# Attention handed over to two dense layers: the last pair's half copies on ScalarE, the third pair's sums and splits moved

## The chip, the cores and the metric

One core of a Trainium2 chip runs the whole program. The metric is the device time of one execution in microseconds (us), as the median of several runs; lower is better. Engines: PE is TensorE (matmuls, PEld its weight loads), DVE is VectorE, ACT is ScalarE, POOL is GpSimd, SP is SyncE, whose queue issues nearly all DMAs.

## The reference

The computation is rotary attention over 4 batches of 8 heads (576 tokens, head size 64), followed by two dense layers on 2304 tokens with model width 512 and hidden width 2048.

```python
q_rot, k_rot = rotate(q), rotate(k)
scores = 1/sqrt(D) * q_rot @ k_rot.T
attn = exp(scores - max); attn = attn / (sum(attn) + 1e-9)
x = attn @ v                        # then heads side by side: 2304 x 512
h = x @ w_in;  g = s * relu(h)**2 + b;  x = g @ w_out
h = x @ w2_in; g = h * sigmoid(1.702 * h); out = g @ w2_out
```

Everything is float32. The kernel feeds PE with a high and a low part of each operand (hi is a rounded copy in the type fp32r, lo is what the rounding left), so each product is three matmuls: hi by hi, lo by hi, hi by lo.

## The kernel before, in words

**Attention.** The 32 heads are worked in 16 pairs. Each engine follows an order written out by hand (`PE_ORDER`, `ACT_ORDER`, `DVE_ORDER`, `POOL_ORDER`, `SP_ORDER`), in which a token such as `sum1@-1` means the job "sum", half 1, of the pair one behind the step. `program` walks through it. The values product `PV` (L714) of a head leaves its result in PSUM as two halves of 64 partitions, one from the high and one from the low part of V. ACT copies one half to the tile `O` (`evac`, L808) and DVE copies the other to `osum` (`half`, L906). POOL's `finish` (L527, L531, L534) adds the two and multiplies by `inv_row`, the inverse row sums, into `xT`. `inv_row` is a single buffer. SP fetches it for a pair from DRAM with three DMAs (`get_inv`, L450), and for the last pair, number 15, only when `x_done` says that pair 14 is finished. For pairs 14 and 15 `finish` runs inside the first step of the layers.

**Layers.** These run in 48 steps (windows) n, 24 for each layer; a step handles 256 hidden columns of one of three chunks of 768 tokens. The input product of a step uses a scheme of 7 block products (`product(n, k)`, L1093, k = 0 to 6), which needs sums of weight blocks (`w_sum`, four POOL additions, L1021, L1022, L1024 and L1026, into the single tile `wsum`) and of the tokens (`x_sum`, POOL). The sums and the raw weights are split: ACT rounds to `win_hi` (`win_high`, L1031 and L1032), POOL takes `win_lo` of the raw part (`win_low`, L1038), DVE that of the sums from step 2 on (`sums_low`, L1042). `wout_high` (ACT, L1253) and `wout_low` (POOL, L1048) split the weights of the output product. The output product of a step is `y_part` (L1121), in three parts for each of its two tiles a and b.

**Within step n.** PE runs products k = 0 to 6 of step n. Between them it puts output parts: behind k = 0, 1, 2 tile b of step n-2, behind k = 3, 4, 5 tile a of step n-1. The seven products share two PSUM banks in turn, so each waits until ACT or DVE has read the one two before it: ACT copies k = 0 to `P1` (`keep_first`, L1137), k = 2 to `U2` (L1226) and k = 3 to `P5` (L1235). DVE adds k = 1 (`block_11`, L1142), k = 4 (L1299, into `h_b`) and k = 5 (L1303, into `h_a`). k = 6 needs the DVE addition of k = 4. For the step before, ACT runs the activation (L1187) and rounds to `ga_hi` and `gb_hi` (L1192); DVE runs the square (L1265 and L1271) and the low parts `ga_lo` and `gb_lo` (L1310). Products k = 0 and 1 of step 0 already run inside attention.

**The order around the change.** Semaphores hold the data; within an engine the order of the program decides. `pool_window(0)` runs `win_low(1)`, `w_sum(2)`, `wout_low(0)`, `finish(14)`, `finish(15)`; `pool_window(1)` begins with `win_low(2)`. Product (2, 0) waits for `win_low(2)` and `sums_low(2)`; the first output part of step n waits for `wout_low(n)` and `ga_lo`. DVE ends attention with the low parts of the first tokens (`xc_lo`, L919) for k = 3 to 6 and then the two half copies of pair 15. ACT in step 0 copies `U2`, `P5`, and then runs `wout_high(0)`, whose raw weights come by a DMA that SP issues once all values products are done. In what follows "(n, k)" is product k of step n.

Of the kernel before, what the change touches and what calls it, by code (L numbers as in the profile page):

```python
# [30 lines left out]
def fused_kernel(nc, q, k, v, w1_in, w1_out, w_s, w_b, w2_in, w2_out,  # L31
# [129 lines left out]
    with outer:  # L161
# [170 lines left out]
        with ExitStack() as ctx:  # L332
# [537 lines left out]
            def attention_vector(dve):  # L870
# [30 lines left out]
                def half(p, h, _):  # L901

                    dve.wait_ge(pv_done, 2 * p + h + 1)
                    if h == 0:
                        need(dve, x_done, p - 1)
                    dve.tensor_copy(osum[p % 2][rows_of(h), :], row(banks("PV", p, h), 0)[rows_of(1 - h), :]).then_inc(half_done, 1)  # L906
# [28 lines left out]
                for n, (first, w) in enumerate(((0, 0), (0, 1), (NM + 1, 0), (NM + 1, 1))):  # L935
# [5 lines left out]
                program(DVE_FIRST, DVE_ORDER, {"max": rowmax, "maxT": rowmaxT, "lo": lo, "loQ": loQ, "loT": loT, "inv": invert, "sum": half,  # L941
                                    "klo": qk_low, "xc": x_low, "first": first_block})

        with ExitStack() as ctx:
# [189 lines left out]
            def keep_first(act, n):  # L1134
                need(act, dve_read, 3 * n - 2)
                act.wait_ge(product_done, 7 * n + 1)
                act.copy(P1[:], hps(n, 0)).then_inc(act_read, 1)  # L1137

            def block_11(dve, n):
                dve.wait_ge(act_read, 4 * n + 1)  # L1140
# [53 lines left out]
            def act_window(act, n):  # L1194
# [3 lines left out]
                if gates:  # L1198
                    act.wait_ge(product_done, 7 * n)
                    act_function(act, a_b[:, 0:N], hps(n - 1, 6), n - 1).then_inc(act_read, 1)  # L1200
                    act.wait_ge(sq_a, n)
                    need(act, y_a, n - 2)
                    g_high(act, ga_hi[(n - 1) % 2][:], a_a[:], n - 1).then_inc(g_hi_a, 1)
                if runs:
                    if n > 0:
                        keep_first(act, n)
                    if j == 0 and C > 0:
                        x_split(act, C, NOPS - 1, True)
                    if splits:
                        x_split(act, C + 1, 0, True)  # L1210
                    if 0 < n and n + 1 < WINDOWS:
                        win_high(act, n + 1)
# [10 lines left out]
                if runs:  # L1223
                    act.wait_ge(product_done, 7 * n + 3)
                    need(act, dve_read, 3 * n)
                    act.copy(U2[:], hps(n, 2)).then_inc(act_read, 1)  # L1226
                    if splits:
# [7 lines left out]
                    act.copy(P5[:], hps(n, 3)).then_inc(act_read, 1)  # L1235
                    if n == 0:
                        wout_high(act, n)
                    if splits:
                        x_split(act, C + 1, 3, True)
                        x_split(act, C + 1, 4, True)  # L1240
# [14 lines left out]
            def dve_window(dve, n):  # L1255
# [4 lines left out]
                if gates:  # L1260
# [3 lines left out]
                    else:  # L1264
                        dve.scalar_tensor_tensor(a_a[:], a_a[:], sb_sb[:, 0:1], a_a[:], ALU.mult, ALU.mult).then_inc(sq_a, 1)  # L1265
                    dve.wait_ge(act_read, 4 * n)
                    if second(m):
# [8 lines left out]
                if runs:  # L1276
# [4 lines left out]
                    if evacuates:  # L1281
                        evacuate(dve, C - 1, 1)
                    if n > 0:
                        block_11(dve, n)
                    if 2 <= n + 1 < WINDOWS:
                        sums_low(dve, n + 1)
# [3 lines left out]
                if runs:  # L1290
# [11 lines left out]
                    dve.wait_ge(product_done, 7 * n + 6)  # L1302
                    dve.tensor_tensor(h_a[:, N:CH], hps(n, 5), U2[:], ALU.add).then_inc(dve_read, 1)  # L1303
                    if splits:
                        x_split(dve, C + 1, 5, False)
# [6 lines left out]
            def pool_window(pool, n):  # L1312
# [3 lines left out]
                if C + 1 < 2 * NCH and 1 <= j <= 4:  # L1316
# [3 lines left out]
                    x_sum(pool, C + 1, j - 1)  # L1320
                if n + 2 < WINDOWS:
                    w_sum(pool, n + 2)
                wout_low(pool, n)
                if n == 0:
                    finish(pool, NPAIR - 2)
                    finish(pool, NPAIR - 1)
# [104 lines left out]
```

## Time and profile before

| what | us |
|---|---|
| median of 3 runs | 1076.78 (1075.91 to 1077.61) |
| the profiled execution, its own time | 1077.13 |
| its span, first to last instruction | 1075.2 |
| PE busy | 1043.3 (97% of the span) |
| DVE, ACT, POOL busy | 737.1, 634.5, 706.5 |
| TensorE clock granted, mean | 0.998 of full speed |

What lies around the span is 1077.13 less 1075.2, 1.9 us. Attention takes up to about 314 us from the start, the 48 steps the rest. Times in the trace are from the start of the span. A row of the timeline gives the start, the duration, the engine, the line and operation, the tile written and those read, and in brackets the idle time before it with what ended it. A matmul lasts longer than the distance to the next one, as they are pipelined.

### The profile page before, as it was taken

How to read it: one execution, taken by the hardware profiler on the slowest of the kernel's cores; microseconds unless marked ns; L12 is line 12 of the kernel's file. 1: busy time of each engine (PE TensorE's matmuls, PEld its weight loads, DVE VectorE, ACT ScalarE, POOL GpSimd, SP SyncE). 2: the span in 40 equal slices, each digit the busy share in tenths (PEclk: the TensorE clock that was granted, in tenths of full speed). 3: DMA queues.
4: the chain of work that ended last, by engine and by line, in shares of the span. 5: the costliest groups of instructions: out<-in, count | busy, mean ns of one | idle time of the engine just before them, and what ended most of it. 6: DMA issues, size and time to landing. Idle time of an engine off the chain costs nothing.

```text
span 1075.2 us, 17071 instructions
## 1 busy us (share of the span) xinstructions
PE 1043.3 (97%) x6234; PEld 962.3 (90%) x6234; DVE 737.1 (69%) x874; ACT 634.5 (59%) x1125; POOL 706.5 (66%) x586
## 2 busy tenths in 40 slices
PE   4899999999989999999999999999999999999998
PEld 4799999999988999999999999998888889888887
DVE  6888888889887757755586564875577555854542
ACT  4887878787865545654565454654456434654542
POOL 6878787878888856667556754766566675555420
PEclk9999999999999999999999999999999999999999
DMA  4555455554232221221212221221222422241101
GB/s 107 129 150 150 111 143 143 153 132 114 65 96 71 79 79 59 79 60 59 78 59 80 60 78 60 59 79 59 79 60 69 128 61 78 59 137 59 60 20 59
DMA packets 100613, 93.03 MB, mean 87 GB/s; under 512 B 15652, under 2 KB 78644, under 8 KB 100532
## 3 DMA queue, kind: packets, MB, share of 16 engines
q1 hardware_dynamic: 99408, 90.94, 29.6%
q8 instruction: 50, 0.82, 0.3%
q10 hardware_dynamic: 1124, 1.02, 0.3%
q14 instruction: 31, 0.25, 0.1%
HBM read 69.44 MB, written 4.79 MB: 69 GB/s over the span
## 4 chain that ended last, share of the span: by engine, by line
PE 83%; POOL 5%; DVE 5%; ACT 3%; DMA 2%; issue 1%; SPq 0%; ACTq 0%; POOLq 0%; DVEq 0%
PE psum L1121 37%; PE psum L1093 31%; PE psum L714 6%; PE psum L642 3%; PE psum L668 3%; ACT E L777 2%; DVE negmax L876 1%; DVE Xlo L886 1%; PE psum L744 1%; DVE osum L906 1%; DVE QK L929 1%; POOL win_lo L1038 1%; POOL xT L531 1%; DMA sin<-in_k_sin_dram 0%; POOL osum L527 0%
## 5 line engine op out<-in xcount | busy, mean ns | idle before, releaser
L1038 POOL TENSOR_TENSOR win_lo<-win_raw,win_hi 128x768 fp32r<-128x768 f32 x48 | 101.6, 2116 | 244.2 <-ACT win_hi L1032 244.2
L1093 PE MATMUL psum<-xc_hi,win_hi 128*128 128x384 f32 x672 | 226.7, 337 | 4.2 <-DVE h_b L1299 2.4
L1093 PE MATMUL psum<-xc_lo,win_hi 128*128 128x384 f32 x672 | 226.7, 337 | 0.0
L1093 PE MATMUL psum<-xc_hi,win_lo 128*128 128x384 f32 x672 | 226.1, 336 | 0.0
L1093 PEld LDWEIGHTS psum<-xc_hi,win_hi 128*128 128x128 f32 x672 | 126.8, 189 | 13.7 <-issue 3.8
L1093 PEld LDWEIGHTS psum<-xc_lo,win_hi 128*128 128x128 f32 x672 | 126.7, 189 | 8.2
L1048 POOL TENSOR_TENSOR wout_lo<-wout_raw,wout_hi 128x1024 fp32r<-128x1024 f32 x48 | 119.6, 2492 | 16.5 <-ACT wout_hi L1253 16.5
L1093 PEld LDWEIGHTS psum<-xc_hi,win_lo 128*128 128x128 f32 x672 | 126.8, 189 | 0.0
L777 ACT ACTIVATE E<-psum,negmax 128x576 f32<-128x576 f32 x128 | 94.6, 744 | 13.4 <-DVE negmax L876 13.3
L876 DVE TENSOR_REDUCE negmax<-psum 128x1 f32<-128x576 f32 x128 | 91.0, 751 | 14.1 <-PE psum L642 13.5
L1042 DVE TENSOR_TENSOR win_lo<-wsum,win_hi 128x1024 fp32r<-128x1024 f32 x46 | 95.1, 2068 | 4.2 <-ACT win_hi L1032 4.1
L1299 DVE TENSOR_TENSOR h_b<-psum,P 128x384 f32<-128x384 f32 x48 | 26.7, 556 | 101.0 <-PE psum L1093 101.0
L642 PE MATMUL psum<-QK,Q 128*128 128x320 f32 (+1 forms) x512 | 85.5, 307 | 9.7 <-ACT E L777 6.7
L886 DVE TENSOR_TENSOR Xlo<-psum,Xhi 128x512 fp32r<-128x512 f32 x128 | 82.7, 681 | 4.8 <-ACT Xhi L791 4.7
L642 PEld LDWEIGHTS psum<-QK,Q 128*128 128x128 f32 x512 | 71.0, 189 | 14.9 <-issue 6.8
L1303 DVE TENSOR_TENSOR h_a<-psum,U 128x384 f32<-128x384 f32 x48 | 26.7, 557 | 82.6 <-PE psum L1093 82.5
L1021 POOL TENSOR_TENSOR wsum<-win_raw 128x256 f32<-128x256 f32 x48 | 63.8, 1328 | 20.3 <-DVE win_lo L1042 18.8
L714 PE MATMUL psum<-Xhi,V 128*128 128x256 f32 (+1 forms) x256 | 70.2, 302 | 0.4 <-DVE XTlo L894 0.4
L668 PE MATMUL psum<-id_sb,E 128*128 128x128 f32 x512 | 70.1, 276 | 0.6 <-ACT E L777 0.3
L791 ACT CAST Xhi<-psum 128x512 fp32r<-128x512 f32 x128 | 69.3, 581 | 0.3 <-PE psum L668 0.2
L714 PE MATMUL psum<-Xlo,V 128*128 128x256 f32 (+1 forms) x256 | 69.5, 296 | 0.0
L1253 ACT CAST wout_hi<-wout_raw 128x1024 fp32r<-128x1024 f32 x48 | 50.6, 1055 | 28.8 <-PE psum L1121 26.2
(154 smaller groups left out, 2852.5 us busy)
## 6 DMA issues: line engine op xcount, KB each, us to landing
wout_raw<-in_moe_w_out_dram SPq DMA_DIRECT2D x48, 512.0 KB, 3.6
win_raw<-in_moe_w_in_dram SPq DMA_DIRECT2D x48, 256.0 KB, 2.8
win_raw<-in_moe_w_in_dram SPq DMA_DIRECT2D x96, 128.0 KB, 2.8
Q<-QK SPq DMA_DIRECT2D x60, 144.0 KB, 2.8
QK<-QK SPq DMA_DIRECT2D x30, 288.0 KB, 3.4
vraw<-in_v_dram SPq DMA_DIRECT2D x32, 128.0 KB, 2.5
raw<-in_q_dram SPq DMA_DIRECT2D x30, 128.0 KB, 2.9
raw<-in_k_dram SPq DMA_DIRECT2D x30, 128.0 KB, 2.7
```

What stands on the lines that cost most here:

```text
L642: mm = pe.matmul(ps[:, a:b], Q[h][p % 2][:, at:at + P], QK[h][p % 2][:, part, c:c + b - a], start=part == 0, stop=part == 1)
L668: mm = pe.transpose(ps[:, t * P:(t + 1) * P], E[p % 2][:, t, h, c:c + P], id_sb[:])
L714: mm = pe.matmul(ps[:, a:b], V[h][:, j, :, :].rearrange("p a d -> p (a d)"), x, start=j == 0 and n == 0, stop=j == NM and n == 1, skip_gro ...
L777: act.activation(E[p % 2][:, j, h, :], row(banks("S", p, h, j), h), ACT.Exp, bias=negmax[p % 2][:, c:c + 1], accum_out=sums[p % 2][:, c:c ...
L791: act.copy(Xhi[:, h, j, 0:MAIN], banks("X", p, h, j)).then_inc(et_hi, 1)
L876: dve.tensor_reduce(negmax[p % 2][:, c:c + 1], row(banks("S", p, h, j), h), AX_X, ALU.max, negate=True).then_inc(max_done, 1)
L886: dve.tensor_tensor(Xlo[:, h, j, 0:MAIN], banks("X", p, h, j), Xhi[:, h, j, 0:MAIN].bitcast(F32), ALU.subtract).then_inc(et_lo, 1)
L1038: pool.tensor_tensor(win_lo[m % 2][:, 0:3 * BLK], win_raw[m % 2][:, 0:3 * BLK], win_hi[m % 2][:, 0:3 * BLK].bitcast(F32), ALU.subtract).th ...
L1042: last = eng.tensor_tensor(win_lo[m % 2][:, 3 * BLK:7 * BLK], wsum[:], win_hi[m % 2][:, 3 * BLK:7 * BLK].bitcast(F32), ALU.subtract)
L1048: pool.tensor_tensor(wout_lo[m % 2][:], wout_raw[m % 2][:], wout_hi[m % 2][:].bitcast(F32), ALU.subtract).then_inc(wout_lo_done, 1)
L1093: mm = pe.matmul(hps(n, k), w[n % 2][:, at:at + P], x[k][:, t, :], start=k in FRESH and t == 0 and i == 0, stop=t == HK - 1 and i == 2, sk ...
L1121: mm = pe.matmul(yps(bank)[:, col:col + size], lhsT, rhs, start=first and col == 0 and i == 0, stop=last and i == 2, skip_group_check=True)
```

## The change

The half copies of pair 15 leave DVE: `half` returns at once for it, and a new `last_halves` has ACT copy both behind `P5` of step 0 and ahead of `wout_high(0)`. On POOL, `w_sum(2)` goes from ahead of `wout_low(0)` to behind it, still ahead of `finish(14)`. In step 1 only, ACT's `keep_first` goes ahead of `ga_hi`, `U2` (now in a function, `keep_third`) ahead of `gb_hi`, and `win_high(2)` from ahead of `gb_hi` to behind `P5`; DVE's `block_11` goes ahead of the square of tile b, and `sums_low(2)` from ahead of `gb_lo` to the end of the step. All other steps keep their order.

```diff
--- before.py
+++ after.py
@@ -900,6 +900,8 @@
 
                 def half(p, h, _):
 
+                    if p == NPAIR - 1:
+                        return
                     dve.wait_ge(pv_done, 2 * p + h + 1)
                     if h == 0:
                         need(dve, x_done, p - 1)
@@ -940,6 +942,13 @@
                 dve.wait_ge(scale_set, 1)
                 program(DVE_FIRST, DVE_ORDER, {"max": rowmax, "maxT": rowmaxT, "lo": lo, "loQ": loQ, "loT": loT, "inv": invert, "sum": half,
                                     "klo": qk_low, "xc": x_low, "first": first_block})
+
+            def last_halves(act):
+
+                p = NPAIR - 1
+                act.wait_ge(x_done, p - 1)
+                for h in range(2):
+                    act.copy(osum[p % 2][rows_of(h), :], row(banks("PV", p, h), 0)[rows_of(1 - h), :]).then_inc(half_done, 1)
 
         with ExitStack() as ctx:
             def sb(name, shape, dt=F32):
@@ -1136,6 +1145,11 @@
                 act.wait_ge(product_done, 7 * n + 1)
                 act.copy(P1[:], hps(n, 0)).then_inc(act_read, 1)
 
+            def keep_third(act, n):
+                act.wait_ge(product_done, 7 * n + 3)
+                need(act, dve_read, 3 * n)
+                act.copy(U2[:], hps(n, 2)).then_inc(act_read, 1)
+
             def block_11(dve, n):
                 dve.wait_ge(act_read, 4 * n + 1)
                 dve.wait_ge(product_done, 7 * n + 2)
@@ -1198,17 +1212,21 @@
                 if gates:
                     act.wait_ge(product_done, 7 * n)
                     act_function(act, a_b[:, 0:N], hps(n - 1, 6), n - 1).then_inc(act_read, 1)
+                    if n == 1:
+                        keep_first(act, n)
                     act.wait_ge(sq_a, n)
                     need(act, y_a, n - 2)
                     g_high(act, ga_hi[(n - 1) % 2][:], a_a[:], n - 1).then_inc(g_hi_a, 1)
                 if runs:
-                    if n > 0:
+                    if n > 1:
                         keep_first(act, n)
+                    if n == 1:
+                        keep_third(act, n)
                     if j == 0 and C > 0:
                         x_split(act, C, NOPS - 1, True)
                     if splits:
                         x_split(act, C + 1, 0, True)
-                    if 0 < n and n + 1 < WINDOWS:
+                    if 1 < n and n + 1 < WINDOWS:
                         win_high(act, n + 1)
                 if gates:
                     act.wait_ge(sq_b, n)
@@ -1221,9 +1239,8 @@
                 if evacuates:
                     evacuate(act, C - 1, 0)
                 if runs:
-                    act.wait_ge(product_done, 7 * n + 3)
-                    need(act, dve_read, 3 * n)
-                    act.copy(U2[:], hps(n, 2)).then_inc(act_read, 1)
+                    if n != 1:
+                        keep_third(act, n)
                     if splits:
                         x_split(act, C + 1, 2, True)
                     if evacuates:
@@ -1234,7 +1251,10 @@
                     act.wait_ge(product_done, 7 * n + 4)
                     act.copy(P5[:], hps(n, 3)).then_inc(act_read, 1)
                     if n == 0:
+                        last_halves(act)
                         wout_high(act, n)
+                    if n == 1:
+                        win_high(act, n + 1)
                     if splits:
                         x_split(act, C + 1, 3, True)
                         x_split(act, C + 1, 4, True)
@@ -1263,6 +1283,8 @@
                         dve.tensor_tensor(a_a[:], h_a[:], a_a[:], ALU.mult).then_inc(sq_a, 1)
                     else:
                         dve.scalar_tensor_tensor(a_a[:], a_a[:], sb_sb[:, 0:1], a_a[:], ALU.mult, ALU.mult).then_inc(sq_a, 1)
+                    if n == 1:
+                        block_11(dve, n)
                     dve.wait_ge(act_read, 4 * n)
                     if second(m):
                         dve.tensor_tensor(a_b[:, 0:N], hps(m, 6), a_b[:, 0:N], ALU.mult).then_inc(last_read, 1)
@@ -1280,9 +1302,9 @@
                         x_split(dve, C + 1, 0, False)
                     if evacuates:
                         evacuate(dve, C - 1, 1)
-                    if n > 0:
+                    if n > 1:
                         block_11(dve, n)
-                    if 2 <= n + 1 < WINDOWS:
+                    if 2 < n + 1 < WINDOWS:
                         sums_low(dve, n + 1)
                 if gates:
                     dve.wait_ge(g_hi_b, n)
@@ -1301,6 +1323,8 @@
                         x_split(dve, C + 1, 4, False)
                     dve.wait_ge(product_done, 7 * n + 6)
                     dve.tensor_tensor(h_a[:, N:CH], hps(n, 5), U2[:], ALU.add).then_inc(dve_read, 1)
+                    if n == 1:
+                        sums_low(dve, n + 1)
                     if splits:
                         x_split(dve, C + 1, 5, False)
 
@@ -1318,10 +1342,11 @@
                         pool.wait_ge(x_lo, NOPS * (C + 1) - POOL_OPS)
                         x_ready(pool, C + 1)
                     x_sum(pool, C + 1, j - 1)
-                if n + 2 < WINDOWS:
+                if 0 < n and n + 2 < WINDOWS:
                     w_sum(pool, n + 2)
                 wout_low(pool, n)
                 if n == 0:
+                    w_sum(pool, n + 2)
                     finish(pool, NPAIR - 2)
                     finish(pool, NPAIR - 1)
```

## Rows read from the trace of the kernel before

**Rows 1.** the page, the chain that ended last, by engine

```profile
PE 83%; POOL 5%; DVE 5%; ACT 3%; DMA 2%; issue 1%; SPq 0%; ACTq 0%; POOLq 0%; DVEq 0%
```

**Rows 2.** waits of PE from 346.3 us to the end

```profile
PE psum L1121 <- POOL wout_lo L1048: 0.2, 1, 0.2
```

**Rows 3.** the chain in order of time (start us, us, what)

```profile
335.20 1.81 POOL win_lo L1038
...
343.87 2.37 POOL wout_lo L1048
...
346.29 1.68 PE psum L1121 x9
```

**Rows 4.** timeline of POOL (start us, us, what, [idle before <-releaser])

```profile
317.16 1.26 POOL L1021 TENSOR_TENSOR wsum<-win_raw 128x256 f32<-128x256 f32 x1
...
321.27 2.37 POOL L1048 TENSOR_TENSOR wout_lo<-wout_raw,wout_hi 128x1024 fp32r<-128x1024 f32 x1
323.60 2.14 POOL L527 TENSOR_TENSOR osum<-osum,O 128x576 f32<-128x576 f32 x1
...
327.67 1.03 POOL L534 TENSOR_TENSOR xT<-osum,inv_row 128x64 f32<-128x64 f32 x1
328.67 1.41 POOL L527 TENSOR_TENSOR osum<-osum,O 128x576 f32<-128x576 f32 x1
333.63 1.30 POOL L531 TENSOR_TENSOR xT<-osum,inv_row 128x512 f32<-128x512 f32 x1 [3.55 <-DMA inv_row<-inv_dram]
```

**Rows 5.** timeline of ACT

```profile
315.08 0.64 ACT L808 COPY O<-psum 64x576 f32<-64x576 f32 x1
...
316.28 0.48 ACT L1235 COPY P<-psum 128x384 f32<-128x384 f32 x1
317.84 1.05 ACT L1253 CAST wout_hi<-wout_raw 128x1024 fp32r<-128x1024 f32 x1 [1.08 <-DMA wout_raw<-in_moe_w_out_dram]
```

**Rows 6.** timeline of DVE

```profile
315.25 2.59 DVE L919 TENSOR_TENSOR xc_lo<-xT,xc_hi 128x768 fp32r<-128x768 f32 x1
317.76 1.49 DVE L919 TENSOR_TENSOR xc_lo<-x_sums,xc_hi 128x768 fp32r<-128x768 f32 x1
319.27 1.54 DVE L906 COPY osum<-psum 64x576 f32<-64x576 f32 x2
320.85 0.56 DVE L1299 TENSOR_TENSOR h_b<-psum,P 128x384 f32<-128x384 f32 x1
...
322.78 1.67 DVE L1265 SCALAR_TENSOR_TENSOR a_a<-a_a,sb_sb 128x768 f32<-128x768 f32 x1 [0.91 <-ACT a_a L1187]
324.38 2.17 DVE L1271 SCALAR_TENSOR_TENSOR a_b<-a_b,sb_sb 128x768 f32<-128x768 f32 x1
326.48 2.04 DVE L1310 SCALAR_TENSOR_TENSOR ga_lo<-a_a,sb_sb,ga_hi 128x768 fp32r<-128x768 f32 x1
```

**Rows 7.** timeline of PE

```profile
321.55 0.48 PE L1093 MATMUL psum<-xc_hi,win_hi 128*128 128x384 f32 x1 [2.35 <-DVE h_b L1299]
...
325.27 0.34 PE L1093 MATMUL psum<-xc_hi,win_hi 128*128 128x384 f32 x1
...
326.31 0.33 PE L1093 MATMUL psum<-xc_hi,win_hi 128*128 128x384 f32 x1
...
329.04 0.45 PE L1093 MATMUL psum<-xc_hi,win_hi 128*128 128x384 f32 x1 [1.52 <-DVE h_a L1142]
...
330.21 0.40 PE L1121 MATMUL psum<-ga_hi,wout_hi 128*128 128x512 f32 x1
...
337.55 0.34 PE L1093 MATMUL psum<-xc_hi,win_hi 128*128 128x384 f32 x1
```

**Rows 8.** durations min/median/max ns, L1022 and L1271 (the columns end in first and last start)

```profile
L1022 POOL TENSOR_TENSOR wsum<-win_raw x47: 723/735/1452, 307.1 to 1020.5; 128x256 f32<-128x256 f32 x47
...
L1271 DVE SCALAR_TENSOR_TENSOR a_b<-a_b,sb_sb x24: 1005/1018/2175, 324.4 to 685.6; 128x768 f32<-128x768 f32 x24
```

**Rows 9.** PE, PEld, DVE, ACT, POOL busy, granted clock, DMA; between 321.5 and 329.0 us

```profile
321.50:329.00 7.50, 5.97 (x24) 5.68 (x24) 6.59 (x6) 6.15 (x10) 7.42 (x5) 0.77 0.00 0
```

## The prediction

> **What bounds the kernel now.** I read the chain that ended last first: PE holds 83% of it [rows 1]. Then the waits of PE behind 346.3 us: there is one in 729 us, of 0.2 us, for `wout_low(1)` [rows 2]. So whatever PE gains or loses by the start of the first output part of step 1, at 346.29 [rows 3], stays to the end, and the change is to be judged by that one moment. Next I asked what sets it. The chain in order of time has POOL work ahead of it: `win_low(2)` at 335.20, then an `x_sum`, `w_sum(3)` and `wout_low(1)`, which ends at 343.87 + 2.37 = 346.24 [rows 3]. `win_low(2)` starts when `finish(15)` ends, and that waited for `inv_row` up to 333.63 [rows 4]. That transfer is issued only when `finish(14)` is over, at 327.67 + 1.03 = 328.70 [rows 4]. POOL runs without a gap from 317.16 to there. PE on the other hand has waits between 319.2 and 329.0: 2.35 us for `h_b` and 1.52 us for `h_a` [rows 7]. They look like the thing to repair, but PE, repaired, meets the POOL chain. At 337.55 it starts (2, 0) [rows 7], only 0.54 us behind the end of `win_low(2)` at 335.20 + 1.81 = 337.01 [rows 3]: PE's slack against POOL there is half a microsecond.
>
> **Part 1, the half copies.** DVE loses two copies, 1.54 us at 319.27 [rows 6]. ACT gets them behind `P5`, which ends at 316.76. They read and write what one `evac` copy does, 64 x 576, so they cost at most 0.64 us each [rows 5], and begin one 0.55 us behind the other as neighbours here overlap a little: 316.8 to 317.95. ACT would otherwise sit idle for 1.08 us up to 317.84, for the DMA of `wout_raw` [rows 5]. So `wout_high(0)` slips by 0.1 us and ends at about 318.95 and not 318.89. Without that cover it would slip by 1.2 us. The new wait of ACT, for pair 13's `finish`, was met inside attention. `finish(15)` needs the halves far later than 318, so nothing waits.
>
> **Part 2, `w_sum(2)` behind `wout_low(0)`.** POOL is free at 317.05, but `wout_low(0)` needs `wout_high(0)`: it stands idle until 319.0, where before it had begun its four additions at 317.16. Behind the start the work up to the end of `finish(14)` is the same: `w_sum` 4 x 0.72, `wout_low` 2.37, `finish` 1.41 + 1.29 + 0.31, 8.3 us when nothing disturbs it (the 0.72 is the shortest of L1022 [rows 8], 2.37 and 1.41 are [rows 4], and the last two together are the 1.57 from 333.63 to 335.20 [rows 3, 4]). It took 328.70 - 317.16 = 11.54. The 3.3 us more go with DVE: in that stretch lie five DVE instructions with two SBUF inputs, at 315.25 (its end), 317.76, 322.78, 324.38 and 326.48, of 1.5 to 2.6 us each [rows 6] where such a one takes 1.01 alone [rows 8]. They interlock with POOL's. The one at 324.38 ends (326.55) 0.8 us behind the end of POOL's L527 (325.74), and POOL's next ones are long by 0.6 to 0.7 us each. That is 3.3 / 5 = 0.66 us of POOL per DVE instruction. After the change DVE has four of them beside this work (L1265, L1271, and L1310 for `ga_lo` and `gb_lo`; the low part at 317.76 now meets an idle POOL, takes about 0.95 us and ends near 318.7). Sum: 319.0 + 8.3 + 4 x 0.66 = 329.95 and not 328.70, **+1.3 us**. Bounds: with no such DVE instruction in the way 327.3 (-1.4), with the stretch as long as before, 319.0 + 11.54 = 330.5 (+1.8).
>
> The Trainium skill, page "SBUF — State Buffer", section "SBUF: two separate sides", says why: the port pair that DVE and GpSimd share is an exclusive lock held for the whole instruction, and the other engine blocks. The trace agrees with the 0.8 us above. By that rule one counts collisions; were it a division of bandwidth one would scale the stretch, and the sum would be 0.5 us larger.
>
> **Part 3, the transfer and `finish(15)`.** SP's three DMAs go out 1.3 us later, so `inv_row` is there at 333.63 + 1.3 = 334.9; SP's loads of later weights behind them slip as much, under the 11 us that POOL needs from one step to the next. DVE is by now 2 to 3 us ahead of its old times, so its L1271 and L1310 of step 2 fall upon `finish(15)`, which had taken its undisturbed 1.57 us: +0.66 to +0.8. `finish(15)` ends near 337.3 where it was 335.20: **+2.1 us**. `win_low(2)` ends at 339.1, and (2, 0) starts at 339.2 and not 337.55: +1.65.
>
> **Part 4, what PE and DVE gain, and why it is hidden.** `h_b` is no longer behind the copies: DVE ends it at 319.3, k = 6 of step 0 follows at once and not at 321.55, and the clock stays up. `block_11(1)` ahead of the square of tile b is done at 323.2, so (1, 3) need not wait. The square of tile b and `ga_lo` follow to about 325.7; the first output part starts at 325.8 where it was 330.21 [rows 7]. From there to (2, 0) PE needs 337.55 - 330.21 = 7.34 us, so it would want (2, 0) at 333.2. There it stands until 339.2, for 6 us. `win_high(2)` (1.8 us on ACT) starts with `w_sum(2)`, near 326.3, and is over before `h_b` of step 1 wants ACT at 329; `sums_low(2)` runs at 331.8 to 333. Neither sets a time. For `keep_first`, `keep_third` and `block_11` the cost is nothing: the same instructions, earlier, on engines that wait there.
>
> **Part 5, the clock.** After 2.35 us of idle PE the matmuls ran at half rate: the twelve from 321.55 took 325.27 - 321.55 = 3.72 us, and six at full rate take 326.31 - 325.27 = 1.04 [rows 7]; the granted clock of that stretch is 0.77 of full [rows 9], between the levels of 1.2 and 2.4 GHz. That spell cost 3.72 - 2.08 = 1.6 us. Before the 1.52 us gap at 329.04 PE was busy as well, and there the rate held. A gap of 6 us should bring the clock down again, and now on the path: **+1.6 us**. Bounds: 0 and, with the spell half as long again, 2.4.
>
> **Part 6, on to 346.29.** From (2, 0) to there PE took 346.29 - 337.55 = 8.74, of which 0.2 was the wait for `wout_low(1)`. POOL, from 339.1, needs `x_sum` 1.8, `w_sum(3)` 2.9 and `wout_low(1)` 2.4 undisturbed, to 346.2. PE comes later, so the 0.2 goes. **Sum: +1.65 + 1.6 - 0.2 = +3.1 us.** Against the profiled execution (span 1075.2 and 1.9 around it, 1077.13) that is 1080.2. The median is 0.35 lower, 1076.78, so I forecast 1079.9.
>
> **Rivals.** A measurement of this kernel can tell about 0.2% from no change, 2.15 us: 1074.6 and 1078.9 are the limits.
> *A, the forecast, 0.60:* `finish(14)` late, PE stands, the clock falls: +3.1; with the bounds above +2.0 to +4.5.
> *B, POOL late but the clock stays up or is back at once, 0.17:* +1.5 (1078.3), from +0.7 to +2.1. For it: most gaps here leave the rate as it was. Against it: the shorter one at 321.55 did not.
> *C, POOL meets one or two DVE instructions fewer, 0.13:* `win_low(2)` ends about where it did, PE starts (2, 0) at 337.5, and the result is 0 with the clock up, +1.4 with it down.
> *D, faster, 0.10:* the idle POOL and the empty DVE keep out of each other's way altogether. Then `finish(14)` ends at 327.3, `finish(15)` at 333.8, (2, 0) starts at 335.7 after a gap of 2.5 us, and `wout_low(1)` is there by 342.9: 335.7 - 337.55 - 0.2 = -2.1 to -2.5 us, 1074.5. It decides from the point at which `finish(14)` ends before 328.7; every microsecond before that is one off the end, unless the clock takes it back. Against it: three of the four DVE instructions depend on PE and ACT only, and fall into the same stretch.
> That the change doesn't do what it says I leave out: the new order on each engine is plain in the diff.
>
> **The numbers.** Slower by over 0.2%: nearly all of A (0.56), a little of B and C (0.05): 0.61. Faster: most of D, 0.08. The rest, 0.31, is within. The range goes from 1076.7, where C without the clock is still in, to 1081.5, the upper end of A with 0.05 left out; below lies D with a part of C. A's own range is 1078.8 to 1081.3.
>
> **What would show it.** Right: k = 6 of step 0 near 319.3; POOL idle for about 1.9 us ahead of `wout_low(0)`; L534 of `finish(14)` ending near 330; PE idle for some 6 us ahead of (2, 0), with the releaser POOL `win_lo`, and matmuls at half rate behind it; the first output part of step 1 near 349. Wrong: `finish(14)` ending before 328.7, (2, 0) before 337.5, or half rate nowhere behind 337.

## The result, and the profile after

The changed kernel takes 1080.41 us (median of 7 runs, 1079.19 to 1081.17) against 1076.78 before on the same chip. The ratio is 1.0031 with a 95% interval of 1.0019 to 1.0043: 3.6 us slower, where I had forecast 3.1 us and 1079.9. The profiled execution took 1080.41, its span is 1078.3 against 1075.2, 3.1 us more.

The PE timeline of the changed kernel (start us, us, what, in brackets the idle time before with its releaser) answers to [rows 7]. Lines behind the edits have moved by 2 to 24: the input product is L1102, the output product L1130.

```profile
319.74 0.41 PE L1102 MATMUL psum<-xc_hi,win_hi 128*128 128x384 f32 x1
...
326.50 0.48 PE L1130 MATMUL psum<-ga_hi,wout_hi 128*128 128x512 f32 x1 [1.29 <-issue]
...
339.40 0.69 PE L1102 MATMUL psum<-xc_hi,win_hi 128*128 128x384 f32 x1 [5.32 <-POOL win_lo L1047]
...
342.96 0.28 PE L1130 MATMUL psum<-gb_lo,wout_hi 128*128 128x256 f32 x1
...
349.51 0.39 PE L1130 MATMUL psum<-ga_hi,wout_hi 128*128 128x512 f32 x1
```

k = 6 of step 0 starts at 319.74 with no wait and not after 2.35 us. The first output part starts at 326.50, where it was 330.21. Then comes what the forecast turned on: (2, 0) stands for 5.32 us, released by POOL's `win_lo`, and the matmuls of 384 columns behind it are spaced 0.32 us and not 0.17. Full rate is back at 342.96. The first output part of step 1 starts at 349.51 and not 346.29. The clock, in the windows view (busy time of PE, PEld, DVE, ACT, POOL, then the granted clock), is at half, the level of 1.2 GHz:

```profile
329.00:337.50 8.50, 5.08 (x29) 4.36 (x27) 6.04 (x6) 2.80 (x4) 5.96 (x7) 0.92 0.33 96
337.50:341.00 3.50, 1.60 (x5) 1.60 (x6) 0.19 (x1) 0.00 (x0) 3.50 (x2) 0.50 0.14 37
```

The POOL timeline answers to [rows 4]:

```profile
319.67 2.40 POOL L1057 TENSOR_TENSOR wout_lo<-wout_raw,wout_hi 128x1024 fp32r<-128x1024 f32 x1 [2.23 <-ACT wout_hi L1273]
322.02 1.45 POOL L1030 TENSOR_TENSOR wsum<-win_raw 128x256 f32<-128x256 f32 x1
...
324.13 1.45 POOL L1033 TENSOR_TENSOR wsum<-wsum,win_raw 128x256 f32<-128x256 f32 x1
325.66 1.33 POOL L1035 TENSOR_TENSOR wsum<-win_raw,wsum 128x256 f32<-128x256 f32 x1
326.95 2.15 POOL L527 TENSOR_TENSOR osum<-osum,O 128x576 f32<-128x576 f32 x1
...
330.44 0.33 POOL L534 TENSOR_TENSOR xT<-osum,inv_row 128x64 f32<-128x64 f32 x1
...
334.61 1.28 POOL L531 TENSOR_TENSOR xT<-osum,inv_row 128x512 f32<-128x512 f32 x1 [2.46 <-DMA inv_row<-inv_dram]
...
336.83 2.51 POOL L1047 TENSOR_TENSOR win_lo<-win_raw,win_hi 128x768 fp32r<-128x768 f32 x1
...
343.96 2.42 POOL L1057 TENSOR_TENSOR wout_lo<-wout_raw,wout_hi 128x1024 fp32r<-128x1024 f32 x1
```

POOL waits 2.23 us for `wout_hi`, then has `wout_low(0)`, the four sums (322.02 to 326.95), `finish(14)` to 330.77, the transfer to 334.61, `finish(15)` to 336.87 and `win_low(2)` to 339.34. `wout_low(1)` ends at 346.38, 3 us ahead of PE. DVE and ACT over the same time answer to [rows 6] and [rows 5]:

```profile
318.18 0.95 DVE L921 TENSOR_TENSOR xc_lo<-x_sums,xc_hi 128x768 fp32r<-128x768 f32 x1
319.05 0.55 DVE L1321 TENSOR_TENSOR h_b<-psum,P 128x384 f32<-128x384 f32 x1
...
321.14 1.74 DVE L1285 SCALAR_TENSOR_TENSOR a_a<-a_a,sb_sb 128x768 f32<-128x768 f32 x1 [0.92 <-ACT a_a L1201]
...
323.68 1.31 DVE L1293 SCALAR_TENSOR_TENSOR a_b<-a_b,sb_sb 128x768 f32<-128x768 f32 x1
324.92 1.48 DVE L1334 SCALAR_TENSOR_TENSOR ga_lo<-a_a,sb_sb,ga_hi 128x768 fp32r<-128x768 f32 x1
326.32 1.49 DVE L1334 SCALAR_TENSOR_TENSOR gb_lo<-a_b,sb_sb,gb_hi 128x768 fp32r<-128x768 f32 x1
```

```profile
317.22 1.29 ACT L951 COPY osum<-psum 64x576 f32<-64x576 f32 x2
318.54 1.05 ACT L1273 CAST wout_hi<-wout_raw 128x1024 fp32r<-128x1024 f32 x1
```

Attention ended 0.44 us later in this execution than in the one of before (last values matmul at 314.21, before at 313.77). That is not the change: over the 13 profiles of this case, this matmul starts anywhere from 313.57 to 314.38. So that kernels can be compared, the table gives three moments counted from that matmul (the mark), in us: the end of `finish(14)`, the start of (2, 0) and the start of the first output part of step 1, and then the difference of the last to the kernel before. In the last column stands the median less that of the kernel before on the same chip, with the interval of the ratio. The moments are those of one profiled execution of each kernel, the medians are of all its executions. Most profiled executions lie within 0.5 us of their median, but that of E2 lies 0.95 us below it and that of E8 1.3 us above, as the slowest of its 11.

| kernel | `finish(14)` ends | (2, 0) | output, step 1 | to before | median to before (ratio, 95%) |
|---|---|---|---|---|---|
| before | 14.9 | 23.8 | 32.5 | | |
| after | 16.6 | 25.2 | 35.3 | +2.8 | +3.6 (1.0019 to 1.0043) |
| E1 halves alone | 15.3 | 23.5 | 32.7 | +0.2 | +0.9 (0.9997 to 1.0015) |
| E2 sums ahead | 15.7 | 24.2 | 33.4 | +0.9 | +2.0 (1.0007 to 1.0025) |
| E3 sums in the transfer | 12.9 | 23.1 | 31.6 | -0.9 | -0.5 (0.9988 to 1.0006) |
| E4 filler | 16.5 | 25.5 | 34.0 | +1.4 | +1.8 (1.0004 to 1.0021) |
| E5 halves back | 15.4 | 25.8 | 34.3 | +1.8 | +1.6 (1.0007 to 1.0024) |
| E6 pad | 18.5 | 26.6 | 36.7 | +4.1 | +4.7 (1.0031 to 1.0055) |
| E7 finish ahead | 7.6 | 21.6 | 30.7 | -1.8 | -1.2 (0.9977 to 0.9994) |
| E8 E7's move on the kernel before | 7.6 | 27.0 | 35.4 | +2.9 | +1.7 (1.0006 to 1.0023) |
| E9 finish in attention | 1.4 | 21.0 | 30.1 | -2.5 | -1.8 (0.9979 to 1.0003) |
| E10 E9's move on the kernel before | 1.4 | 25.1 | 33.4 | +0.9 | +0.9 (0.9996 to 1.0014) |
| E11 after, again | 16.6 | 25.2 | 36.3 | +3.8 | +4.1 (1.0023 to 1.0049) |

### The profile page after: what moved, and what is told of

Its sections match the earlier page's. It is cut to its first block, busy times and chain, and to the rows that moved or that the text cites. A ratio compares the mean times of both kernels' runs of the same rounds, so it can differ in the third digit from the quotient of the medians.

```text
span 1078.3 us, 17070 instructions
## 1 busy us (share of the span) xinstructions
PE 1045.1 (97%) x6234; PEld 963.6 (89%) x6234; DVE 730.4 (68%) x872; ACT 636.9 (59%) x1127; POOL 703.3 (65%) x586
## 4 chain that ended last, share of the span: by engine, by line
PE 85%; POOL 4%; DVE 4%; ACT 3%; issue 2%; DMA 1%; SPq 0%; ACTq 0%; POOLq 0%; DVEq 0%
PE psum L1130 37%; PE psum L1102 31%; PE psum L714 6%; PE psum L668 4%; PE psum L642 4%; ACT E L777 2%; DVE negmax L876 1%; PE psum L744 1%; DVE osum L908 1%; DVE Xlo L886 1%; POOL win_lo L1047 1%; POOL xT L531 0%; PE psum L678 0%; POOL osum L527 0%; PE psum L694 0%
## 5 line engine op out<-in xcount | busy, mean ns | idle before, releaser
L1102 PE MATMUL psum<-xc_hi,win_hi 128*128 128x384 f32 x672 | 226.4, 337 | 5.8 <-POOL win_lo L1047 5.3
L1102 PE MATMUL psum<-xc_lo,win_hi 128*128 128x384 f32 x672 | 226.2, 337 | 0.0
L1102 PE MATMUL psum<-xc_hi,win_lo 128*128 128x384 f32 x672 | 225.6, 336 | 0.0
L1102 PEld LDWEIGHTS psum<-xc_hi,win_hi 128*128 128x128 f32 x672 | 126.4, 188 | 15.3 <-POOL win_lo L1047 5.6
L1102 PEld LDWEIGHTS psum<-xc_lo,win_hi 128*128 128x128 f32 x672 | 126.5, 188 | 8.2
L1102 PEld LDWEIGHTS psum<-xc_hi,win_lo 128*128 128x128 f32 x672 | 126.4, 188 | 0.0
L777 ACT ACTIVATE E<-psum,negmax 128x576 f32<-128x576 f32 x128 | 94.7, 745 | 13.5 <-DVE negmax L876 13.3
L1051 DVE TENSOR_TENSOR win_lo<-wsum,win_hi 128x1024 fp32r<-128x1024 f32 x46 | 94.7, 2059 | 1.9 <-ACT win_hi L1041 1.7
```

The source lines that it names most:

```text
L777: act.activation(E[p % 2][:, j, h, :], row(banks("S", p, h, j), h), ACT.Exp, bias=negmax[p % 2][:, c:c + 1], accum_out=sums[p % 2][:, c:c ...
L1051: last = eng.tensor_tensor(win_lo[m % 2][:, 3 * BLK:7 * BLK], wsum[:], win_hi[m % 2][:, 3 * BLK:7 * BLK].bitcast(F32), ALU.subtract)
L1102: mm = pe.matmul(hps(n, k), w[n % 2][:, at:at + P], x[k][:, t, :], start=k in FRESH and t == 0 and i == 0, stop=t == HK - 1 and i == 2, sk ...
```

## The experiments

Theory: POOL's chain (`finish(14)`, transfer, `finish(15)`, `win_low(2)`) sets (2, 0); moving the sums behind `wout_low(0)` lengthened it, and the gap that PE's own gain opened brought the clock down on the path. Rivals: the steps moved on ACT and DVE are the cause, or there is no slack-free chain on POOL at all. Part 1 is, as in the prediction, the half copies on ACT, and part 2 the place of the sums on POOL. What is left of the change are the moves in step 1.

**E1, part 1 alone.** The kernel before, with `half` returning for the last pair and `last_halves` on ACT.

```diff
                 def half(p, h, _):
+                    if p == NPAIR - 1:
+                        return
...
                     if n == 0:
+                        last_halves(act)
                         wout_high(act, n)
```

> The kernel before with part 1 alone (half copies of pair 15 on ScalarE). POOL-chain theory: k = 6 of step 0 starts 1.5 to 2 us earlier and no longer at half rate, but POOL still begins its four additions near 317.2, finish(14) still ends near 328.7, and (2, 0) cannot start before win_low(2) ends near 337: the time is that of before within 1 us. Rival (the waits of PE for DVE set the end): 1.6 to 3 us faster than before.

Measured +0.9 us, not told from no change. The waits of PE show where the 2.35 us went (E1, PE timeline):

```profile
319.33 0.41 PE L1102 MATMUL psum<-xc_hi,win_hi 128*128 128x384 f32 x1 [0.64 <-DVE h_b L1309]
...
327.30 0.45 PE L1102 MATMUL psum<-xc_hi,win_hi 128*128 128x384 f32 x1 [2.96 <-DVE h_a L1151]
...
346.60 0.50 PE L1130 MATMUL psum<-ga_hi,wout_hi 128*128 128x512 f32 x1 [0.56 <-POOL wout_lo L1057]
```

The wait for `h_b` is 0.64 us and the rate holds behind it, but 2.96 us are now lost on `h_a` of `block_11(1)`, and half rate follows there from 328.9 on. PE then starts (2, 0) at 337.38, when `win_low(2)` has just ended (337.33), and ahead of 346.60 it waits 0.56 us for `wout_lo`. So part of what part 1 gains is lost in the next wait for DVE, and POOL takes the rest. The rival, a kernel 1.6 to 3 us faster, is out.

**E2, part 2 undone.** The changed kernel with the sums back ahead of `wout_low(0)`.

```diff
-                if 0 < n and n + 2 < WINDOWS:
+                if n + 2 < WINDOWS:
                     w_sum(pool, n + 2)
                 wout_low(pool, n)
                 if n == 0:
-                    w_sum(pool, n + 2)
                     finish(pool, NPAIR - 2)
```

> The changed kernel with the sums of the third pair back ahead of wout_low(0). POOL-chain theory: POOL's 2.2 us of idle go, finish(14) ends about 1.3 us earlier than in the changed kernel, (2, 0) starts 1 to 2 us earlier, behind a gap of about 4 us that still brings the clock down: 1 to 2 us faster than the changed kernel, still 0.5 to 2.5 us slower than before. Rival (the place of the sums on POOL is innocent, the loss comes from the steps moved on ScalarE and VectorE): the same as the changed kernel, some 3.5 us slower than before.

1078.95 us, +2.0 against +3.6 for the change: in the range of the theory, so the place of the sums accounts for nearly half of the loss. (The two intervals overlap a little. In the table `finish(14)` ends 0.9 us and (2, 0) starts 1.0 us earlier than in the changed kernel.) The rest comes with the steps that stayed moved: DVE's squares come earlier and fall upon `wout_low(0)`, which takes 3.12 us and not 2.37, and `finish(14)` still ends 0.7 us later than before. E2 is E1 with the moves in step 1, on the same chip, and takes 1.1 us more (0.7 in the table). So with part 1 in place these moves gain nothing. The difference is within the intervals, and no run undoes them alone in the changed kernel. The expectation had one thing wrong. The gap ahead of (2, 0) is 1.43 us, not 4, and the half rate lies elsewhere, behind the gap ahead of the first output part (E2, PE timeline and windows):

```profile
327.31 0.76 PE L1130 MATMUL psum<-ga_hi,wout_hi 128*128 128x512 f32 x1 [2.08 <-issue]
...
337.85 0.45 PE L1102 MATMUL psum<-xc_hi,win_hi 128*128 128x384 f32 x1 [1.43 <-POOL win_lo L1047]
```

```profile
327.00:331.00 4.00, 3.69 (x13) 3.44 (x14) 2.17 (x2) 2.08 (x4) 3.72 (x3) 0.57 0.07 13
```

There it costs PE time that POOL's chain hides, as (2, 0) still has to wait for `win_lo`.

**E3, the sums in the transfer.** The changed kernel with `w_sum(2)` between the two finishes.

```diff
                 if n == 0:
+                    finish(pool, NPAIR - 2)
                     w_sum(pool, n + 2)
-                    finish(pool, NPAIR - 2)
                     finish(pool, NPAIR - 1)
```

> The changed kernel with the sums of the third pair behind finish(14), in the time in which POOL waits for inv_row. POOL-chain theory: finish(14) ends near 326, inv_row lands near 331, finish(15) ends near 332.5, win_low(2) near 335, (2, 0) starts near 335 behind a gap of 1 to 2 us that leaves the clock up: about 2.5 us faster than before (1 to 3.5), 6 us faster than the changed kernel. Rival (ScalarE, held up by the later sums at win_high(2), is late with the activations of step 1 and takes the gain): no faster than before.

Against the changed kernel 4 us are won back, against before only 0.5, which is no difference: the main number was missed, and the time is the one that the rival gave. The POOL timeline says why:

```profile
319.84 2.40 POOL L1057 TENSOR_TENSOR wout_lo<-wout_raw,wout_hi 128x1024 fp32r<-128x1024 f32 x1 [2.22 <-ACT wout_hi L1273]
322.19 2.15 POOL L527 TENSOR_TENSOR osum<-osum,O 128x576 f32<-128x576 f32 x1
...
330.88 1.44 POOL L527 TENSOR_TENSOR osum<-osum,O 128x576 f32<-128x576 f32 x1
...
334.92 2.51 POOL L1047 TENSOR_TENSOR win_lo<-win_raw,win_hi 128x768 fp32r<-128x768 f32 x1
```

`finish(14)` now ends at 327.29, 12.9 behind the mark, but POOL has no wait left after 319.84: the transfer is hidden, and what sets (2, 0) is the plain amount of work between `wout_hi` and `win_low(2)`, 17.6 us with its collisions (`finish(14)` 5.1 us where it takes 3.0 undisturbed, `win_low(2)` 2.51 where it takes 1.85). I had left the collisions out of this expectation, though the prediction's own rule of 0.66 us each was at hand. ACT was indeed held for 3.5 us at `win_high(2)`, as the rival had it, but what released (2, 0) was POOL's `win_lo`, and the first output part of step 1 had no wait at all. So the rival's number came by another path.

**E4, PE kept busy in the gap.** Ahead of (2, 0) of the changed kernel:

```diff
+                if n == 2 and k == 0:
+                    pe.wait_ge(dve_read, 3 * n)
+                    for i in range(28):
+                        pe.matmul(hps(n, k), xc_hi[0][:, 0, 0:P], xc_hi[0][:, 0, :], start=True, stop=True, skip_group_check=True)
```

> The changed kernel with 28 idle matmuls of 384 columns (4.9 us at full rate) put into the gap ahead of (2, 0), into the PSUM bank that (2, 0) clears at its start. Theory that the half rate behind the gap is on the path: (2, 0) starts when it did, the matmuls behind it run at full rate, and the time is 1.4 to 1.8 us below that of the changed kernel. Rival (POOL's wout_low(1) or ScalarE would set the first output part of step 1 anyway): no gain, the wait comes back ahead of that part.

1078.79, 1.6 us below the changed kernel's first median, though in another set of runs (each against its own kernel before: +1.8 and +3.6); on the marks 35.3 - 34.0 = 1.3, with (2, 0) 0.3 later. E4's windows, from (2, 0) on (compare 337.50:341.00 above, clock 0.50):

```profile
339.40:348.00 8.60, 8.57 (x49) 8.04 (x50) 2.61 (x3) 4.35 (x6) 8.52 (x7) 1.00 0.31 70
```

Between (2, 0) and the output part lie 8.5 us here, 10.1 in the changed kernel. Eight of its 11 executions have a mean clock of 1.000. Work that computes nothing makes the kernel faster: the half rate behind the gap is on the path and costs 1.6 us.

**E5, part 1 undone.** The changed kernel with the half copies back on DVE (the diff of E1 reversed).

> The changed kernel with the half copies of pair 15 back on VectorE. POOL-chain theory: h_b and k = 6 of step 0 come some 1.3 us later than in the changed kernel, but wout_low(0) and the sums keep their place and (2, 0) starts within 1 us of 339, behind a gap of about 4 us instead of 5.3: the time is that of the changed kernel within 1 us (1079.5 to 1081.5). Rival (part 1 is worth its 1.5 us at the end too): 1.3 to 3 us slower than the changed kernel.

1078.35: 2 us *faster* than the changed kernel (1.0 us by the marks; the two intervals overlap a little), outside what both theories said. Two things show in the trace. POOL: ACT begins `wout_high(0)` 4.0 us behind the mark and not 4.3, and then DVE's first square, later by 1.5 us, meets POOL less: the four sums take 3.6 us and not 4.9 and `finish(14)` ends 1.2 us earlier. PE: with a gap of 1.80 us for `h_b` and one of 2.60 us ahead of the first output part (at 328.88) the clock falls at about 330, before (2, 0) and not behind it, and what then releases (2, 0) is DVE's `sums_low(2)`, which ends at 339.29, while `win_low(2)` was done at 336.41 (E5, DVE and PE):

```profile
336.41 2.88 DVE L1049 TENSOR_TENSOR win_lo<-wsum,win_hi 128x1024 fp32r<-128x1024 f32 x1
```

```profile
328.88 0.47 PE L1128 MATMUL psum<-ga_hi,wout_hi 128*128 128x512 f32 x1 [2.60 <-issue]
...
330.94 0.52 PE L1100 MATMUL psum<-xc_lo,win_hi 128*128 128x384 f32 x1
...
339.39 0.41 PE L1100 MATMUL psum<-xc_hi,win_hi 128*128 128x384 f32 x1 [1.39 <-issue]
```

So in the changed kernel part 1 is not worth nothing but costs: it brings DVE's work into POOL's, and it makes PE's gap one long one in the worst place.

**E6, POOL loaded.** The changed kernel with this ahead of `finish(14)`:

```diff
+        pad = keep("pad", [P, 768])
...
+                    for i in range(2):
+                        pool.tensor_tensor(pad[:, i * 384:(i + 1) * 384], win_raw[0][:, 0:384], win_raw[0][:, 512:896], ALU.add)
                     finish(pool, NPAIR - 2)
```

> The changed kernel with two additions of 384 elements on GpSimd (about 1.0 us each, into a tile of their own) ahead of finish(14). POOL-chain theory: they are on the path, finish(14), the transfer, win_low(2) and (2, 0) all slip by 2.0 us (1.3 to 2.7, as collisions with VectorE shift), and so does the time: about 1082.5. Rival (GpSimd has slack there): no change.

`finish(14)` ends 1.9 us later, (2, 0) and the output part 1.4 us later (by the marks), the median is 1081.52, 1.1 above the changed kernel's. The intervals overlap, but all five executions (1081.32 and more) lie above all 12 of the changed kernel (1081.25 at most, E11 included). Of the 1.9 us, 1.4 arrive and not all: `win_low(2)`, pushed away from DVE's work, takes 1.80 us and not 2.51. POOL is on the path; the rival is out. Its gap (E6, PE timeline):

```profile
340.49 0.69 PE L1103 MATMUL psum<-xc_hi,win_hi 128*128 128x384 f32 x1 [6.65 <-POOL win_lo L1048]
```

**E7, `finish(14)` where POOL sat idle.** The changed kernel with

```diff
+                if n == 0:
+                    finish(pool, NPAIR - 2)
                 wout_low(pool, n)
                 if n == 0:
                     w_sum(pool, n + 2)
-                    finish(pool, NPAIR - 2)
                     finish(pool, NPAIR - 1)
```

> The changed kernel with finish(14) ahead of wout_low(0), where GpSimd sat idle; the sums stay behind wout_low(0). POOL-chain theory: the transfer of inv_row is over before finish(15) wants it, GpSimd works without a gap from 317 to win_low(2), 13.1 us of undisturbed work and some 5 us of collisions, (2, 0) starts near 335.3 behind a short gap with the clock up: 2.0 to 2.8 us faster than before, near 1074.6. Rival (collisions on the port now delay VectorE's last xc_lo and take it back on TensorE): no faster than 1 us below before.

1075.61, 1.2 us below before (interval 0.6 to 2.5), 5 us below the changed kernel. Less than the theory's 2.0 to 2.8 and just beyond the rival's 1: both have a share. (2, 0) starts 2.1 us earlier than before, near the 335.3 that I gave (335.64, with attention 0.2 us later); but DVE's last `xc_lo` takes 2.18 us beside `finish(14)` and not 0.95, so PE waits 1.35 us for `h_b` (E7, DVE and PE):

```profile
317.99 2.18 DVE L921 TENSOR_TENSOR xc_lo<-x_sums,xc_hi 128x768 fp32r<-128x768 f32 x1
```

```profile
320.78 0.41 PE L1102 MATMUL psum<-xc_hi,win_hi 128*128 128x384 f32 x1 [1.35 <-DVE h_b L1321]
...
335.64 0.41 PE L1102 MATMUL psum<-xc_hi,win_hi 128*128 128x384 f32 x1 [0.38 <-issue]
...
344.70 0.50 PE L1130 MATMUL psum<-ga_hi,wout_hi 128*128 128x512 f32 x1 [0.45 <-POOL wout_lo L1057]
```

**E8, the same move on the kernel before.**

> The kernel before with finish(14) ahead of w_sum(2) and wout_low(0), and nothing of the change. Theory that the moves on ScalarE and VectorE pay once GpSimd's chain is out of their way, and not without: here TensorE still stands 2.4 us for h_b, falls to half rate, and wants (2, 0) near 337.5 whatever GpSimd does: the time is that of before within 0.7 us, and 2 us above the previous kernel. Rival (the place of finish(14) alone gives the gain): as fast as the previous kernel, 2 us or more below before.

1.7 us *slower* than before (interval 0.6 to 2.5), beyond what was expected, and 2.9 us above E7. POOL's chain is short here, POOL even waits 3.9 us ahead of 346.2. But its work now stands beside DVE's, for which PE waits: the square of tile b takes 3.03 us where it takes 1.0, and PE waits 3.04 and 2.59 us, with half rate behind the first at once and behind the second from 332.3 on (E8, DVE and PE):

```profile
325.21 3.03 DVE L1271 SCALAR_TENSOR_TENSOR a_b<-a_b,sb_sb 128x768 f32<-128x768 f32 x1
```

```profile
322.38 0.66 PE L1093 MATMUL psum<-xc_hi,win_hi 128*128 128x384 f32 x1 [3.04 <-DVE h_b L1299]
...
330.84 0.44 PE L1093 MATMUL psum<-xc_hi,win_hi 128*128 128x384 f32 x1 [2.59 <-DVE h_a L1142]
```

So the change is worth 2.9 us (1078.51 against 1075.61) once `finish(14)` is out of the way, and the early `finish(14)` alone is worth less than nothing. Each needs the other. How the 2.9 us divide between the moves on ACT and DVE and the place of the sums, which differs too, no run shows.

**E9 and E10, `finish(14)` in attention.** On the changed kernel (E9) and on the kernel before (E10): `finish_pair` runs `finish` for `p < NPAIR - 1` and not `- 2`, and the call in `pool_window` goes.

```diff
-                    if p < NPAIR - 2:
+                    if p < NPAIR - 1:
                         finish(pool, p)
...
-                    finish(pool, NPAIR - 2)
```

> The changed kernel with finish(14) at its regular place in attention, behind w_sum(1), where GpSimd waits 2 us for win_hi; it is gone from the layers. POOL-chain theory: GpSimd's work up to win_low(2) loses 3 to 5 us, win_low(1) ends about 1 us later (318) and hides ScalarE's wout_high(0), finish(15) ends near 329.5 and win_low(2) near 332, before TensorE wants it; (2, 0) starts at 333.5 to 334.5 with the clock up: 3 to 4 us faster than before, near 1073.2. Rival (the collisions with VectorE's last xc_lo and with sums_low(2) cost on TensorE what the chain gives, as when finish(14) went ahead of wout_low(0)): 1 to 2 us faster than before.

> The kernel before with finish(14) at its regular place in attention, and nothing of the change. Theory that the moves of the change pay once GpSimd's chain is out of the way: TensorE still stands over 2 us for h_b and falls to half rate, and wants (2, 0) near 337.5: the time is that of before within 1 us, 3 us above the previous kernel. Rival (the early finish(14) alone gives the gain): 2 us or more below before.

E9 takes 1074.85, 1.8 us below before and 5.9 below the changed kernel on the same chip (E11); its interval to before, 0.9979 to 1.0003, just reaches 1. Its 11 executions fall in two groups by the mean granted clock: eight at 0.999 to 1.000 took 1074.5 to 1074.9, three at 0.995 to 0.997 took 1078.1 to 1079.7. The loss fits the clock: by an estimate from these means, 0.997 over 1075 us leaves out 3.2 us of full rate and 0.995 leaves out 5.4 us, and the three are 3.2 to 4.9 us above the median. Where their clock fell is not recorded, as the profile is that of one of the eight. 1.8 us is what the rival gave (1 to 2), not the 3 to 4 us of the theory, though (2, 0) starts at 334.73, near the 333.5 to 334.5 expected. POOL works without a pause from 309.98 on, and `win_low(1)` and DVE's `xc_lo` collide (L1051 3.10 us where it takes 2.40, DVE's L921 3.14 where it takes 0.95); `wout_low(1)` still holds PE for 0.45 us (E9, POOL and PE):

```profile
309.98 2.15 POOL L527 TENSOR_TENSOR osum<-osum,O 128x576 f32<-128x576 f32 x1
...
315.07 3.10 POOL L1051 TENSOR_TENSOR win_lo<-wsum,win_hi 128x1024 fp32r<-128x1024 f32 x1
```

```profile
319.61 0.41 PE L1102 MATMUL psum<-xc_hi,win_hi 128*128 128x384 f32 x1 [0.94 <-DVE h_b L1321]
...
334.73 0.41 PE L1102 MATMUL psum<-xc_hi,win_hi 128*128 128x384 f32 x1 [0.38 <-issue]
...
343.79 0.50 PE L1130 MATMUL psum<-ga_hi,wout_hi 128*128 128x512 f32 x1 [0.45 <-POOL wout_lo L1057]
```

E10 is at +0.9, not told from before, as expected: the early `finish(14)` without the change gives nothing. (2, 0) even starts 1.3 us later by the marks, behind waits of 2.63 and 2.29 us for DVE. E9 is 2.7 us faster than E10 on the same chip, much as E7 is than E8.

**E11, the changed kernel again,** on the chip of E9 and E10.

> The changed kernel once more, on the same chip as the two before it, unchanged: 2 to 4.5 us slower than before if the first result holds; within 1 us of before if that was the chip.

1080.75, +4.1 (interval 2.5 to 5.3): the first result holds. More of the work falls in the spell at half rate. From (2, 0) to the output part it took 11.1 us and not 10.1, with the clock at 0.50 and 0.64 (E11, windows):

```profile
339.00:342.00 3.00, 2.90 (x8) 2.75 (x9) 0.00 (x0) 0.48 (x1) 3.00 (x4) 0.50 0.53 150
342.00:346.00 4.00, 4.00 (x17) 3.75 (x16) 0.40 (x1) 2.25 (x3) 3.92 (x4) 0.64 0.07 21
```

The gap is the same 5.32 us, but the clock falls at another point of it. In the first profile it falls just behind 336.0, more than 3 us ahead of (2, 0), in E11 just behind 338.0, 1 us ahead of it (the changed kernel first, then E11, windows):

```profile
336.00:336.50 0.50, 0.00 (x0) 0.00 (x0) 0.50 (x1) 0.00 (x0) 0.50 (x1) 0.61 0.00 0
```

```profile
338.00:338.50 0.50, 0.00 (x0) 0.00 (x0) 0.00 (x0) 0.00 (x0) 0.50 (x1) 0.57 0.00 0
```

It is back at full rate at 342.96 there and near 344.9 here. So the first execution spent more of its half-rate time idle, where it costs nothing, and the price of one and the same gap is 1.6 us in one execution and 2.5 in the other.

## Why the prediction was right

The forecast was that POOL's chain grows and that PE's gain turns into a gap that costs clock. The two profiled executions differ by 3.28 us, of which 0.44 arose in attention and 2.8 behind it. Term by term, counted from the end of attention:

| step | forecast | measured |
|---|---|---|
| `wout_high(0)` slips | 0.1 | 0.3 |
| end of `finish(14)` | +1.3 | +1.6 |
| `inv_row` there | +1.3 | +0.5 |
| `finish(15)` | +0.7 to +0.8 | +0.7 |
| `win_low(2)` | 0 | +0.7 |
| (2, 0) | +1.65 | +1.4 |
| half rate | +1.6 | +1.6 (E11: 2.5) |
| wait for `wout_low(1)` gone | -0.2 | -0.2 |
| first output part of step 1 | +3.1 | +2.8 (E11: 3.8) |

*Part 1.* The copies follow each other at 0.66 us, not 0.55: 1.29 us for two, so `wout_high(0)` slips by 0.3. Pricing the move at nothing beyond that was wrong in a larger way: E5 has it cost about 2 us in this kernel (1.0 between the profiles). The prediction counted four collisions and their place without asking what they would be with part 1 left out.

*Part 2.* Right in mechanism. From 319.67 to 330.77 are 11.1 us, where the sum gave 8.3 + 4 x 0.66 = 10.94. The count of four collisions holds: four POOL instructions in that stretch are long by 0.6 to 0.7 us each, at 322.02, 324.13, 325.66 and 326.95. E2 shows the price of the place by itself, 1.0 us at (2, 0), and E6 that work on POOL there is on the path.

*Part 3.* Two errors that nearly cancel. From the end of `finish(14)` to the multiplication of `finish(15)` (L531) it took 3.84 us and not 4.93; from the issue of the third DMA to its landing 2.50 us in the chain where it was 3.59 (chain of before, then of the changed kernel):

```profile
329.91 3.59 DMA inv_row<-inv_dram
```

```profile
331.98 2.50 DMA inv_row<-inv_dram
```

Why was not tried; in the six other profiles in which POOL waits there the whole is 3.8 to 4.8. Against it stands one collision more, on `win_low(2)` (2.51 us).

*Part 4.* Right: 319.3, 325.8 and 333.2 were forecast for k = 6, the first output part and the end of step 1; with the 0.44 taken off they came at 319.3, 326.1 and 333.6.

*Part 5.* Right in kind and size: 10.11 us from 339.40 to 349.51 against the 8.54 that I had taken for full rate is 1.57 (E10, without a wait there, has 8.37). E4 shows it by itself. The size has some luck in it: E11, the same kernel, has 2.5, just beyond the bound of 2.4, as the clock falls later in the gap.

*The rivals.* B is out: in both profiles of the changed kernel the clock behind the gap is 0.50, and in none of its 12 executions (7, and 5 of E11) was the mean above 0.998, while with the filler of E4 it was 1.000 in 8 of 11. The mean alone would not show it: most executions of the kernel before have 0.997 or 0.998 too, in its profile by the half rate behind 321.55 [rows 7], which lies ahead of POOL's release. C and D are out with a `finish(14)` that ended 1.6 us later. D's logic, that every microsecond before 328.7 is one off the end, was too simple: E3, E7 and E9 had it earlier by 2, 7 and 13.5 us and gained 0.5, 1.2 and 1.8 us, because then the amount of POOL's work, and DVE beside it, sets the end.

## What to carry to other kernels

When an engine far from the bound feeds the bound by one chain, ask of every reordering what it does to the start of that chain, above all where a step is put behind a wait on another engine: here 2.2 us of new idle on GpSimd moved the release by more than a microsecond, and nothing of the 4 us that TensorE had won ahead of it was left. A gain ahead of a fixed release becomes a gap, and half rate behind that gap adds a cost of its own, 1.6 to 2.5 us here; removing the release and making the gain pay only together (E7 against E8). Where VectorE and GpSimd both read two operands from SBUF, count the collisions one by one, on both engines.

## What the runs showed of the hardware

- Idle matmuls in a gap of 5.3 us made the kernel faster (E4). Without them the first ten behind it ran at half rate: those of 384 columns were spaced 0.32 us and not 0.17, those of 512 columns 0.42 us and not 0.23.
- Which gap brings the clock down does not follow from its length alone. Behind one of 2.08 us (E2) the rate was halved at once, behind one of 2.96 us (E1) only 1.6 us after PE had resumed, behind one of 2.70 us (E3) not at all. In two executions of the changed kernel the clock falls 2 us apart within the same gap, and equal executions of E9 differ by 3 to 5 us with it. I had not expected so large a part of the spread between executions to be the clock.
- A collision of DVE and POOL costs both: the same `xc_lo` of 768 elements took 0.95 us beside an idle POOL (after), 1.49 [rows 6], 2.18 (E7) and 3.14 (E9). The one of 3.14 us starts at 315.85, while POOL's L1051 is running, and ends 0.8 us behind that one's end at 318.17: as it takes 0.95 us alone, it stood for most of POOL's instruction.
